# First x rows loaded by column halves around the reciprocals' spread, and one step's values split ahead of the queries

## The reference

```python
# 1. block-causal attention, q, k, v: (4, 8, 576, 64), block 64
scores = (1 / sqrt(64)) * q @ k.T
scores = where(pos_i // 64 >= pos_j // 64, scores, -1e9)
attn = exp(scores - max); attn = attn / (sum(attn) + 1e-9)
x = attn @ v                                  # as (2304, 512)
# 2. mixture of 4 experts, w1: (4, 512, 1024), w2: (4, 1024, 512)
p = domain_probs / (sum + 1e-9)
x = sum_e p[:, e] * (relu(x @ w1[e]) @ w2[e])
# 3. one more layer: h = x @ w_in; solu = h * softmax(h)
out = (layer_norm(solu) * g_ln) @ w_out
```

## Time and profile before

| | us |
|---|---|
| median of 3 runs (lowest, highest) | 1150.38 (1150.2, 1152.32) |
| the profiled execution's own time | 1152.51 |
| its span, first to last instruction | 1150.7 |
| TensorE busy | 1135.1 |
| VectorE, ScalarE, GpSimd busy | 634.8, 427.7, 418.3 |

### The profile page before, as it was taken

How to read it: one execution, slowest core, us unless ns; L and a number is a source line. 1 busy time by engine, 2 the same in 40 slices (tenths; PEclk the granted TensorE clock), 3 DMA queues, 4 the chain that set the end, 5 groups by cost and what they waited for, 6 DMA issues and landing times.

```text
span 1150.7 us, 16750 instructions
## 1 busy us (share of the span) xinstructions
PE 1135.1 (99%) x6131; PEld 1019.5 (89%) x6131; DVE 634.8 (55%) x1139; ACT 427.7 (37%) x943; POOL 418.3 (36%) x403
## 2 busy tenths in 40 slices
PE   8999999999999999999999999999999999999998
PEld 7999998888999989899998989999998987888887
DVE  7999997444343524343533334453424478667765
ACT  7988885313233211123221113321112354433432
POOL 8998996618145000024300004400003373532330
PEclk9999999999999999999999999999999999999999
DMA  4676768984825122252304071503125100000000
GB/s 153 211 220 216 224 203 251 354 322 152 307 84 197 39 109 84 83 201 99 148 4 188 1 245 59 222 5 142 51 85 199 39 17 10 29 19 28 19 28 37
DMA packets 68342, 146.29 MB, mean 127 GB/s; under 512 B 6064, under 2 KB 34736, under 8 KB 68272
## 3 DMA queue, kind: packets, MB, share of 16 engines
q1 hardware_dynamic: 68272, 145.36, 36.3%
HBM read 114.60 MB, written 30.74 MB: 126 GB/s over the span
## 4 chain that ended last, share of the span: by engine, by line
PE 89%; DMA 5%; DVE 2%; ACT 2%; POOL 1%; SPq 1%; issue 1%; DVEq 0%; ACTq 0%; POOLq 0%
PE s L1748 36%; PE outp L1609 19%; PE s L1609 15%; PE ring L1609 11%; PE ring L1620 3%; DMA x_stash<-x_tmp 2%; PE outp L1655 2%; PE outp L1654 2%; PE ring L1879 1%; DMA work<-in_moe_w 1%; DMA r_scratch<-rt_sb 1%; DMA xr<-x_stash 1%; POOL x_tmp L787 1%; PE s L1822 1%; ACT pr L924 1%
## 5 line engine op out<-in xcount | busy, mean ns | idle before, releaser
L1748 PE MATMUL s<-xr,w1s 128*128 128x384 f32 x2016 | 360.0, 337 | 3.6 <-DVE u L1437 1.7
L1748 PEld LDWEIGHTS s<-xr,w1s 128*128 128x128 f32 x2016 | 350.5, 188 | 9.0 <-DVE u L1437 2.7
L1079 ACT ACTIVATE hid_h<-u 128x384 fp32r<-128x384 f32 x96 | 50.5, 526 | 372.7 <-DVE u L1432 346.0
L722 POOL TENSOR_TENSOR work<-work 128x256 f32<-128x256 f32 x20 | 14.8, 739 | 392.9 <-DMA work<-in_moe_w 267.2
L1387 DVE SCALAR_TENSOR_TENSOR hid_l<-s,hid_h 128x384 fp32r<-128x384 f32 x48 | 26.8, 557 | 125.6 <-ACT hid_h L1075 125.5
L1345 DVE TENSOR_TENSOR u<-s,m_b 128x384 f32<-128x384 f32 x24 | 13.4, 558 | 132.1 <-PE s L1748 132.1
L1748 PE MATMUL s<-w1s,yop_h 128*128 128x512 f32 x252 | 85.2, 398 | 0.4 <-issue 0.3
L1075 ACT ACTIVATE hid_h<-s 128x384 fp32r<-128x384 f32 x48 | 23.6, 491 | 154.7 <-PE s L1609 154.7
L1609 PE MATMUL s<-k_h,qb 128*128 128x288 f32 (+8 forms) x320 | 75.4, 323 | 2.9 <-DVE k_l L1241 1.9
L924 ACT ACTIVATE pr<-s,neg_max 128x576 f32<-128x576 f32 (+2 forms) x144 | 75.8, 538 | 2.1 <-DVE neg_max L1229 1.9
L1609 PE MATMUL outp<-w_h,hid_h 128*128 128x512 f32 x192 | 75.5, 393 | 0.0
(11 more groups left out here) (172 smaller groups left out, 2452.3 us busy)
## 6 DMA issues: line engine op xcount, KB each, us to landing
xr<-x_stash SPq DMA_DIRECT2D x77, 768.0 KB, 6.1
r_sb<-r_scratch SPq DMA_DIRECT2D x16, 576.0 KB, 4.2
x_rows<-x_n SPq DMA_DIRECT2D x32, 288.0 KB, 4.6
work<-x_rows SPq DMA_DIRECT2D x24, 384.0 KB, 5.7
x_stash<-x_tmp SPq DMA_DIRECT2D x12, 768.0 KB, 3.7
work<-in_moe_w SPq DMA_DIRECT2D x32, 256.0 KB, 4.0
stage<-in_moe_w SPq DMA_DIRECT2D x32, 256.0 KB, 5.2
x_stash<-xr SPq DMA_DIRECT2D x7, 768.0 KB, 9.7
```

The source lines that it names most:

```text
L722: pool.tensor_tensor(s1, a21, a22, ALU.add).then_inc(w1_sums, 1)
L1079: act.activation(hid[slot][0][:, :], source, ACT.Relu).then_inc(hid_high, 1)
L1748: last = pe.matmul(target, x, y, start=start and i == 0, stop=stop and i == 2, skip_group_check=True)
```

## The change

```diff
-        x_loaded = sem("x_loaded")
+        x_loaded = [sem(f"x_loaded{h}") for h in range(2)]
...
-            def load_x(sg, t, parts=(0, 1)):
+            def load_x(sg, t, parts=(0, 1), columns=(0, 1)):
...
-                    for h in range(2):
+                    for h in columns:
                         c = z * DC + 2 * h + t
                         sp.dma_start(rows[:, h * 2 * GROUP:(h + 1) * 2 * GROUP],
-                                     x_dram[...]).then_inc(x_loaded, 16)
+                                     x_dram[...]).then_inc(x_loaded[h], 16)
...
                 if p == 9:
-                    load_x(0, 0)
+                    load_x(0, 0, columns=(0,))
...
                 store_r(p)
                 spread_r(p)
+                if p == 9:
+                    load_x(0, 0, columns=(1,))
...
             def x_join(sg, t):
                 i = 2 * sg + t
-                pool.wait_ge(x_loaded, 64 * (i + 1))
...
-                for c0 in range(0, SLOT, 512):
-                    last = pool.tensor_tensor(joined[:, c0:c0 + 512], ..., ALU.add)
+                for h in range(2):
+                    pool.wait_ge(x_loaded[h], 32 * (i + 1))
+                    cols = slice(h * 2 * GROUP, (h + 1) * 2 * GROUP)
+                    last = pool.tensor_tensor(joined[:, cols], x_top[:, cols], x_bottom[:, cols], ALU.add)
...
-                if p == 13:
+                if p in (7, 13):
                     split_values(p)
                     pool.wait_ge(v_split, p + 1)
                 if p + 2 < PAIRS:
                     split_query(p + 2)
-                if p != 13:
+                if p not in (7, 13):
                     split_values(p)
```

More of the change, by code:

```diff
@@ L546, in load_x @@
                     rows = x_bottom if z else x_top
-                    for h in range(2):
+                    for h in columns:
                         c = z * DC + 2 * h + t
                         sp.dma_start(rows[:, h * 2 * GROUP:(h + 1) * 2 * GROUP],
-                                     x_dram[c * P:(c + 1) * P, sg * 2 * GROUP:(sg + 1) * 2 * GROUP]).then_inc(x_loaded, 16)
+                                     x_dram[c * P:(c + 1) * P, sg * 2 * GROUP:(sg + 1) * 2 * GROUP]).then_inc(x_loaded[h], 16)
             def stash_round(sg, t, r):
@@ L761, in x_join @@
                 joined = x_source(sg)[0]
-                for c0 in range(0, SLOT, 512):
-                    last = pool.tensor_tensor(joined[:, c0:c0 + 512], x_top[:, c0:c0 + 512], x_bottom[:, c0:c0 + 512], ALU.add)
+                for h in range(2):
+                    pool.wait_ge(x_loaded[h], 32 * (i + 1))
+                    cols = slice(h * 2 * GROUP, (h + 1) * 2 * GROUP)
+                    last = pool.tensor_tensor(joined[:, cols], x_top[:, cols], x_bottom[:, cols], ALU.add)
                 last.then_inc(x_added, 1)
```

## The result

| | before | changed |
|---|---|---|
| median of 11 runs, us | 1150.38 | 1154.05 |
| lowest, highest | 1148.7, 1152.32 | 1152.35, 1156.44 |
| span of the profiled execution | 1150.7 | 1154.7 |
| ratio, 95% interval | | 1.0032 (1.0024 to 1.0040) |

The change makes the kernel 0.32% slower, 3.7 us. The time lies in the stated range (1148.5 to 1154.5) with 0.45 us to spare, but not where the forecast put it: 1151.7, with 1150.2 to 1152.9 as its own range, and "no change that can be told" with 0.60 (slower had 0.30).

The account below looks back on a forecast made before the run. TensorE, busy 1135.1 of 1150.7 us, was taken as the bound. The terms 2.3 - 1.0 + 1.25 - 1.2 = +1.35 us gave 1151.7 us against the median of 1150.38, range 1148.5 to 1154.5.

Parts of the forecast that it names:

- What bounds it: Whole kernel: TensorE busy 1135.1 of 1150.7 us; GpSimd's slack in steps 8, 10, 11 only 1.65, 1.15, 0.5 us.
- The swap: Step 7, values ahead of queries: GpSimd idles until about 92.9, TensorE stands ahead of `all_right(8)` in step 8, +2.3 us.
- The reciprocals: Step 10: with half the load behind the spread, the reciprocals of step 9 are no longer late, -1.0 us.
- The second half: Step 10: the load's second half lands at 124.7, GpSimd ends the values at 133.4, TensorE waits, +1.25 us.
- Step 11 costs nothing: TensorE stands 0.65 us ahead of `all_right(11)`, covered by 0.63 us it idles anyway before the next scores.
- The joins: `x_join(1, 0)` in two instructions ends sooner, so the queue of stores begins 1.2 us sooner: -1.2 us, between 0 and -2.75.
- the forecast's own sign of being wrong: Step 8 has no idle in TensorE, or the chain of stores keeps its length although it starts sooner.
- Rival 4: Granted clock falls to 1.2 GHz after step 8's idle, rest of the step takes 3.1 us more: 1154.8 us; chance 0.08.
- rival 1: Step 10: the load's second half lands later than 124.7; at 126.7 the time is 1153.7 us; chance 0.20.

Follow-up runs that it names:

- both controls: The changed kernel with TensorE's steps 8 to 11 written out instead of looped, without filler transposes, run twice: 1155.72 and 1156.00 us.

## Why the prediction was half right

- **What bounds it.** Right: the loss is made in steps 8 to 10, where GpSimd had 1.15 to 1.65 us of slack, at the two products named.
- **The swap, +2.3 us.** The mechanism was right, GpSimd idle behind `values_left(6)` and TensorE behind L714; the size was 1.73 (1.69 alone). GpSimd's idle was 2.70 us, not 3.9: it was released at 92.2, 0.5 us sooner than in the trace before, and was free only at 89.5, 0.5 us later. The queries behind the wait took 94.66 to 99.04 = 4.4 instead of 4.86 us. What the forecast didn't say is that this term isn't independent: without it the second half costs 3.02 us, with it 1.75.
- **The reciprocals, -1.0.** Right: write 2.1 us, no wait in step 10. No kernel here came out faster by it, since each way to it moved a wait.
- **The second half, +1.25.** It landed just ahead of 124.38 (forecast 124.7), the join ended at 126.2 (126.6), the values at 133.0 (133.4). That the landing was met is partly luck, as two errors cancel: the spread was issued at 117.11 instead of 118.6, since the first half went out at 110.60 and not at 113.4, and the half landed 7.2 us behind that instead of 6.1. The figures of the Trainium skill (DMA: Bandwidth & Descriptors, Anatomy of one DMA), given for GpSimd's path, make it 5.2 us by estimate, farther off. TensorE was there at 131.35, 0.8 us sooner than forecast, because step 8 had started 1 us sooner than forecast; so it stood 1.75 us.
- **Step 11 costs nothing.** Its 0.65 us did not appear: no wait ahead of `all_right(11)`, and the 0.63 us idle ahead of the next scores shrank to 0.24.
- **The joins, -1.2.** The term that failed first. SyncE's gap ahead of `load_x(1, 1)` did shrink, from 1.28 to 0.85 us here and to 0.11 with the joins alone. The wrong step is the next one, that "the whole queue of stores begins 1.2 us sooner": the first store waits for ScalarE's cast, which stands behind an operation that waits for TensorE, and not for the join. The store round was not shorter either (11.02 us against 10.50). The chain that ended last leads from it over the second round to ScalarE's cast and to `u`, whose wait grew to 2.31 us. That is the forecast's own sign of being wrong, a chain of stores that keeps its length. The wait for the reload is gone from this profile.
- **Rival 4, the clock, 0.08.** The step that was undervalued. It was a rival on its own, with step 8 as its place and 3.1 us as its price. It came on top of the waits, in 5 of 11 executions; in the profiled one at step 10 and behind the wait for `u`. By the products' starts it cost 3.83 - 2.25 = 1.6 us in step 10, about half of that price, because the clock came back within the step. The row that spoke against it (1.00 in all windows, with idle up to 1.6 us) was taken as a proof, while the new waits of 1.7 to 2.3 us lay outside of what it showed.

The terms of the attention add up to 1.73 + 1.75 - 1.0 = 2.5 us, near the forecast's 2.55, and the executions with a clock of 1.000 lose 1153.3 - 1150.4 = 2.9. So two steps failed: the joins' -1.2, which would have brought 2.55 to 1.35, and the clock, which lifts the loss from 2.9 to 3.7 us in the median. The time of rival 1 (1153.7) came near the measured one by chance, since its condition, a landing behind 125.65, did not occur.

The Trainium skill (TensorE: Matmul & The Clock Gate, Part 1) ties the fall to idle stretches. This case agrees with that, and has 1.69 us of idle ahead of the shortest of them (both controls, step 8), 1.75, 2.06 and 2.31 us ahead of others. These are shorter than the gaps that its rule warns of; here the measurement decides.

## What to carry to other kernels

Where every engine is nearly full, a step moved out of one queue's way has to be paid in the next one's: list the slack of each engine at each point that it feeds, and expect gains smaller than that slack to be handed on. Before you count a gap that closes as time won, follow the chain behind it to the wait that ends last there: SyncE's gap closed, and the stores hung on ScalarE. Put an instruction first only where its input is ready when the engine comes free. And, by what this case shows of waits of 1.7 us and more, count a new idle stretch of TensorE twice, once for the wait and once for a part of the executions in which the work behind it runs at half the clock.

## What the runs showed of the hardware that was not expected

- The granted clock fell from 1.00 to 0.50 behind a single idle stretch of 1.75 us (1.69 us in the controls) in a stage in which TensorE is otherwise at work all the time, in a part of the executions only. With work that nobody needs in such stretches the mean clock was 1.000 in 7 of 7 executions, without it below 1.000 in 5 of 5.
- With four of TensorE's steps written out instead of looped the clock fell in 9 of 10 executions, against 5 of 11 with the loop. That is too few to call it shown, and no cause was tried.
